# Attention steps of three units (one head pair) in place of two, one distance table, and queries scaled on the chip

## What is computed

```python
scores = scale * np.matmul(q, k.transpose(0, 1, 3, 2))
keep = is_global | is_local
dist = np.where(is_global & ~is_local, float(n_local), np.abs(rel).astype(np.float32))
bias = -slopes[:, None, None] * dist[None, :, :]
scores = np.where(keep, scores + bias, -1000000000.0)
a = np.exp(scores - max(scores))
a = a / (sum(a) + 1e-09)
x = np.matmul(a, v)
h = np.maximum(x @ w_in, 0.0)      # first product of the next layer
```

## Time and profile before

| what | value |
|---|---|
| median of 3 runs | 374.99 us |
| the profiled execution's own time | 374.08 us |
| its span, first to last instruction | 372.0 us |
| TensorE busy with matmuls | 361.2 us, 97% |
| VectorE, ScalarE, GpSimd busy | 214.7, 176.6, 76.2 us |
| TensorE in the chain that ended last | 91% of the span |
| mean granted TensorE clock | 0.998 of full |

### The profile page before, as it was taken

One profiled execution on the slowest core, in us unless ns is written; L12 is line 12 of the kernel. 1 busy time (PEld: TensorE's weight loads), 2 busy tenths in 40 slices (PEclk: granted clock), 3 DMA queues, 4 the chain that ended last, 5 costly groups with the idle time before them and its releaser, 6 DMA issues.

```text
span 372.0 us, 6143 instructions
## 1 busy us (share of the span) xinstructions
PE 361.2 (97%) x2266; PEld 323.9 (87%) x2266; DVE 214.7 (58%) x568; ACT 176.6 (47%) x450; POOL 76.2 (20%) x152
## 2 busy tenths in 40 slices
PE   6798999999999999999999999999999999999995
PEld 3466888888888899999988999998899999998884
DVE  5798586767677678679957690213863444441000
ACT  4798575674756469664255650213563111112121
POOL 4859963223233100000020210001410000000000
PEclk9999999999999999999999999999999999999999
DMA  7923323142302304131100000001141000001322
GB/s 234 409 112 130 102 86 127 35 154 84 125 37 70 131 0 169 62 112 56 58 0 0 3 0 0 2 0 45 56 168 60 0 2 0 0 2 58 114 86 90
DMA packets 11796, 27.69 MB, mean 74 GB/s; under 512 B 1520, under 2 KB 3568, under 8 KB 11760
## 3 DMA queue, kind: packets, MB, share of 16 engines
q1 hardware_dynamic: 11328, 26.95, 20.6%
q10 hardware_dynamic: 432, 0.28, 0.2%
HBM read 24.08 MB, written 3.15 MB: 73 GB/s over the span
## 4 chain that ended last, share of the span: by engine, by line
PE 91%; ACT 3%; DVE 3%; DMA 1%; POOL 1%; issue 1%; DVEq 0%; ACTq 0%
PE bank L1502 19%; PE bank L1504 19%; PE bank L1503 19%; PE bank L1471 19%; PE bank L1447 5%; PE bank L1425 4%; PE bank L1404 4%; ACT p_sb L683 2%; DMA counts<-in_n_keys 1%; DVE p_sb L1004 1%; DVE denom L1013 0%; POOL p_sb L588 0%; DVE dist L980 0%; ACT pt_sb L691 0%; POOL bias L576 0%
## 5 line engine op out<-in xcount | busy, mean ns | idle before, releaser
L1471 PE MATMUL bank<-xT,w_hi 128*128 128x384 f32 x256 | 71.3, 348 | 0.0
L588 POOL TENSOR_SCALAR p_sb<-p_sb,denom 128x256 f32<-128x256 f32 (+1 forms) x96 | 44.3, 481 | 53.3 <-DVE denom L1015 53.1
L1471 PEld LDWEIGHTS bank<-xT,w_hi 128*128 128x128 f32 x256 | 45.6, 188 | 3.5 <-issue 2.5
L683 ACT ACTIVATE p_sb<-p_sb,row_min 128x256 f32<-128x256 f32 (+1 forms) x96 | 46.3, 486 | 2.2 <-DVE row_min L1004 2.0
L1471 PE MATMUL bank<-xT,w_lo 128*128 128x384 f32 x128 | 44.6, 348 | 0.0
L1502 PE MATMUL bank<-g_hi,w_hi 128*128 128x386 f32 (+1 forms) x128 | 43.3, 338 | 0.0
L1504 PE MATMUL bank<-g_hi,w_lo 128*128 128x386 f32 (+1 forms) x128 | 43.2, 337 | 0.0
L1503 PE MATMUL bank<-g_lo,w_hi 128*128 128x386 f32 (+1 forms) x128 | 43.1, 337 | 0.0
L1041 DVE SCALAR_TENSOR_TENSOR c_sb<-h_sb,conv_sb,c_sb 128x382 f32<-128x382 f32 (+1 forms) x64 | 40.2, 628 | 2.3
L691 ACT COPY pt_sb<-bank 128x512 f32<-128x512 f32 (+1 forms) x41 | 22.6, 552 | 36.7 <-PE bank L1425 36.7
L1004 DVE CUSTOM_DVE_ANT_0 p_sb<-bank,bias 128x256 f32<-128x256 f32 (+1 forms) x96 | 33.1, 399 | 3.6 <-PE bank L1404 2.9
(11 more groups left out here) (96 smaller groups left out, 750.4 us busy)
## 6 DMA issues: line engine op xcount, KB each, us to landing
stage<-in_weights SPq DMA_DIRECT2D x17, 512.0 KB, 3.2
v_sb<-in_v SPq DMA_DIRECT2D x8, 390.0 KB, 3.1
k_sb<-in_k SPq DMA_DIRECT2D x8, 384.0 KB, 3.4
out_dram<-out_sb SPq DMA_DIRECT2D x12, 256.0 KB, 2.0
q_sb<-in_q SPq DMA_DIRECT2D x14, 192.0 KB, 2.5
k_sb<-in_k SPq DMA_DIRECT2D x6, 256.0 KB, 3.4
v_sb<-in_v SPq DMA_DIRECT2D x5, 260.0 KB, 2.7
stage_late<-in_weights SPq DMA_DIRECT2D x2, 512.0 KB, 12.5
```

The costliest lines, as they stand in the source:

```text
L588: nc.gpsimd.tensor_scalar(probs_h, probs_h, denom[:, u % SLOTS, h:h + 1], 1.0, ALU.mult, ALU.mult).then_inc(scaled, 1)
L683: nc.scalar.activation(p_sb[:, u % SLOTS, h, 0:n], p_sb[:, u % SLOTS, h, 0:n], ACT.Exp, bias=row_min[:, u % SLOTS, h:h + 1], scale=-1.0, a ...
L1471: last = nc.tensor.matmul(banks[5 + j % 3][:, 0:C], w, x, start=r == 0, stop=r == F1_GROUP - 1)
```

## The change

TensorE's loop takes one triple at a time: turn three units with 8 matmuls of `f1` behind each, then the scores of the triple two ahead in one block (three units), then `weigh` of this triple's three units. `f1` starts with triple 4, which is unit 12; 12 triples hold 24 matmuls each, again 288. The banks change: `weigh` has bank 4 alone, so `weigh` of a triple waits until `rest_of_x` of the triple before has read it; transposes have bank 3 alone after unit 12, and `pt_sb` three slots for four; `f1` has banks 6 and 7 until its last 96 matmuls. ScalarE and VectorE follow in loops by triples. VectorE copies 6 of the first 12 transposed units.

One table of distances of 640 columns stands for the eight of `bias`; it is built in three parts between the first units. The slope of a head comes in as the scale of the VectorE instruction, and so the queries are multiplied by a factor per head pair beforehand: GpSimd does that, 17 instructions, from factors that 8 short VectorE memsets write. All pieces of the weights of `f1` are split by GpSimd, 8 in place of 6.

```diff
-PT_SLOTS = 4
+PT_SLOTS = TG
-F1_FIRST = GU + 2
-F1_STEP = 8
+F1_FIRST = HP
+F1_STEP = 24
+PIECES_AFTER = {8: 1, 11: 1, 14: 2, 17: 2, 20: 2}
...
+        def score_cols(u, h):
+            p, tt = divmod(u, TG)
+            bank = banks[(2, 5)[h] if tt == 2 else (6, 7)[h] if p == 1 else h]
+            at_col = tt % 2 * 2 * P
+            return bank[:, at_col:at_col + keys(u)]
...
+            def scale_queries(pg):
+                queries = q_sb[:, pg % 2, :]
+                pool.wait_ge(q_in[pg % 2], 16 * (pg // 2 - 1))
+                nc.gpsimd.tensor_scalar(queries, queries, q_scale[:, pg % HP:pg % HP + 1], 1.0, ALU.mult, ALU.mult
+                                        ).then_inc(q_scaled, 1)
...
+            pieces = 0
             for u in range(ALL_UNITS):
                 scale_probs(u)
-                if u in (1, 2, 4, 5):
-                    table(4 + u // 2 + u // 5)
-                if PIECE_FIRST <= u < PIECE_FIRST + (NW1 - 1) * PIECES:
-                    split_piece(u - PIECE_FIRST)
+                if u == 1:
+                    scale_first_queries(2, slice(0, C), q_rest, True)
+                if u == 4:
+                    scale_first_queries(3, slice(0, C), q_rest, True)
+                for pg in range(HP, ALL_TRIPLES):
+                    if scale_unit(pg) == u:
+                        scale_queries(pg)
+                for _ in range(PIECES_AFTER.get(u, 0)):
+                    split_piece(pieces)
+                    pieces += 1
...
+            soften(0)
+            soften(1)
+            copy_pt(0)
+            soften(2)
+            for p in range(ALL_TRIPLES):
+                u = TG * p
+                for tt in range(TG):
+                    if p + 1 < ALL_TRIPLES:
+                        soften(u + TG + tt)
+                    if p >= F1_FIRST and tt == 2:
+                        relu_h(2 * (p - F1_FIRST))
+                    if u + tt > 0 and not turned_on_dve(u + tt):
+                        copy_pt(u + tt)
+                    if tt == 0 and p > 0:
+                        round_x(p - 1)
+                if p >= F1_FIRST:
+                    relu_h(2 * (p - F1_FIRST) + 1)
+            round_x(ALL_TRIPLES - 1)
...
+            for p in range(1, ALL_TRIPLES + 1):
+                u = TG * p
+                for tt in range(TG):
+                    if p + 1 < ALL_TRIPLES:
+                        bias_scores(u + TG + tt)
+                    if tt > 0 and p < HP and turned_on_dve(u + tt):
+                        take_pt(u + tt)
+                rest_of_x(p - 1)
...
+                if p > F1_FIRST:
+                    taps(*divmod(2 * (p - 1 - F1_FIRST), KF))
+                if p < HP:
+                    invert_sums(u + TG, 2)
+                    invert_sums(u + TG + 2, 1)
+                elif p + 1 < ALL_TRIPLES:
+                    invert_sums(u + TG, TG)
+                if p > F1_FIRST:
+                    taps(*divmod(2 * (p - 1 - F1_FIRST) + 1, KF))
...
             def turn_probs(u):
...
+                if u > GU and u % TG:
                     wait_pt(pe, u - 1)
-                    wait_pt(pe, u - 2)
...
+            for p in range(ALL_TRIPLES):
+                for tt in range(TG):
+                    turn_probs(TG * p + tt)
+                    if p == 0 and tt == 1:
+                        third_scores(1)
+                    if p >= F1_FIRST:
+                        for _ in range(F1_STEP // TG):
+                            f1(f1_next)
+                            f1_next += 1
+                if p + 2 < ALL_TRIPLES:
+                    scores(p + 2)
+                for tt in range(TG):
+                    weigh(TG * p + tt)
```

More of the change, by code:

```diff
@@ L382, in turned_on_dve, with copies @@
         def turned_on_dve(u):
-            return u < F1_FIRST and u % 2 == 1
+            return u < GU and (u % TG == 1 or u % TG == 2 and u // TG % 2 == 1)
+        def copies(u, on_dve):
+            return sum(turned_on_dve(i) == on_dve for i in range(u + 1))
         def wait_pt(eng, u):
             if turned_on_dve(u):
-                eng.wait_ge(pt_in_odd, u // 2 + 1)
+                eng.wait_ge(pt_in_dve, copies(u, True))
             else:
-                eng.wait_ge(pt_in, u // 2 + 1 if u < F1_FIRST else u + 1 - F1_FIRST // 2)
+                eng.wait_ge(pt_in, copies(u, False))
         def staged(n):
@@ L399, in wait_chunk @@
                 eng.wait_ge(chunk_in[n % 2], 16 * (n // 2))
+        INVERTED_ALONE = (0, 1, 2, 5, 8, 11, 14)
         def inversion(u):
[L403 to L412, removed]
+            if u < TG * (HP + 1):
+                return sum(i <= u for i in INVERTED_ALONE) - 1 + sum(i <= u for i in range(TG, TG * (HP + 1), TG))
+            return len(INVERTED_ALONE) + HP + u // TG - (HP + 1)
         def values_of(u):
@@ L1402, in score @@
-                for h in range(2):
-                    rows = slice(h * D, (h + 1) * D)
-                    last = nc.tensor.matmul(score_bank(u, h)[:, u % 2 * 2 * P:u % 2 * 2 * P + n],
-                                            queries[rows, tt * P:(tt + 1) * P], keys_t[rows, at_key:at_key + n],
-                                            start=True, stop=True)
-                return last
-            def scores(u):
-                wait_if(pe, biased, 2 * u - (4 if u < F1_FIRST else 0))
-                score(u)
-                score(u + 1).then_inc(scored, 1)
@@ L1415, in turn_probs @@
-            def turn_probs(u):
-                if u < F1_FIRST and u >= 2:
-                    wait_pt(pe, u - 2)
-                if u >= F1_FIRST:
+                else:
+                    queries, keys_t = q_sb[:, u // TG % 2, :], k_sb[:, u // TG % 2, :]
+                rows = slice(h * D, (h + 1) * D)
+                return nc.tensor.matmul(score_cols(u, h), queries[rows, tt * P:(tt + 1) * P],
+                                        keys_t[rows, at_key:at_key + n], start=True, stop=True)
@@ new lines, in score_unit, with scores @@
+            def score_unit(u):
+                score(u, 0)
+                return score(u, 1)
+            def scores(p):
+                u = TG * p
+                if p == 0:
+                    pe.wait_ge(k_first, 16)
+                elif p < HP:
+                    pe.wait_ge(k_second if p == 1 else k_rest, 16)
+                else:
+                    pe.wait_ge(k_in[p % 2], 16 * (p // 2 - 1))
+                pe.wait_ge(q_scaled, queries_scaled(p, 0))
+                if p >= 2:
+                    pe.wait_ge(biased, 2 * (TG * p - 1 if p > 2 else 2))
+                score_unit(u)
+                last = score_unit(u + 1)
+                if p < 2:
+                    last.then_inc(scored_first, 1)
+                if p != 1:
+                    third_scores(p)
@@ L1470, in f1 @@
                 x = xT[:, kappa % 2, (0, 1, 0)[part], kk, :]
-                last = nc.tensor.matmul(banks[5 + j % 3][:, 0:C], w, x, start=r == 0, stop=r == F1_GROUP - 1)
+                last = nc.tensor.matmul(h_bank(j)[:, 0:C], w, x, start=r == 0, stop=r == F1_GROUP - 1)
                 if r == F1_GROUP - 1:
```

253 lines of the change are left out of this document (101 added, 152 removed).

## The result

| what | before | after |
|---|---|---|
| median of 8 runs each | 375.12 us (373.98 to 376.02) | 373.19 us (371.74 to 374.23) |
| ratio of the times, 95% interval | | 0.9955 [0.9936, 0.9974] |
| the profiled execution: own time, span | 374.08, 372.0 us | 373.0, 371.2 us |
| TensorE busy with matmuls | 361.2 us | 359.6 us |
| VectorE, ScalarE, GpSimd busy | 214.7, 176.6, 76.2 us | 215.2, 176.8, 89.5 us |

A forecast was written before the change was run, and what follows sets the result against it. Softmax engines pace the units before the first `f1`; then TensorE's block columns and changes cost. 374.08 - 1.8 (first part) - 1.7 (filler phase) + 0.1 = 370.7 us profiled, 371.6 median; range 368.6 to 374.8.

The forecast's parts named there:

- The filler phase: First `f1` to last 96: fewer changes between blocks, net 1.7 us saved, 99.6 to 97.9.
- the change from `weigh` straight to transposes: TensorE's new block change in each triple: 0.06 us taken, 12 times, 0.7; bounds 0 and 0.10.
- The rule of the Trainium skill: Alternative price for block changes: all equally dear, 0.19 us each, 3.0 saved in place of 3.5.
- The first part: Start of the kernel up to the first `f1`: 34.56 to 32.8, 1.8 us saved.
- Then I walk the lists: Engines' instruction lists followed before the filler: pace no better, filler from unit 12 not 14, first `f1` at 32.8, 1.8 us saved.
- the loop: Before the filler: inversion, GpSimd, queries, transposes, copy, scores, `rest_of_x`, inversions; 5.2 to 5.8 us a triple.
- The start gives nothing: Rival: GpSimd's pieces and queries delay triples, first `f1` at 34.8, total 373.6; chance 0.20, shared with blocks giving nothing.
- A shorter start: Rival: shorter loop and hidden table, first `f1` at 30.1 to 31, total 368.9; chance 0.18.
- Slower: one bank for transposes: Rival: filler-phase second and third transposes wait for the copy before, 24 times 0.25 us, total 377.6; chance 0.12.
- What would show it: Signs in the trace: first `f1` at 32.8, no idle marks behind it, last 96 from 130.8, `weigh` 1.24 to 1.45.

The follow-up runs named there:

- The split of blocks: Changed kernel with four of the third unit's eight `f1` matmuls moved between scores and `weigh` of a triple: 375.43 us, ratio 1.0013 to the kernel before.
- the gaps filled: Changed kernel plus 11 matmuls on zeros into bank 4, six behind triple 1's scores, five behind the first transposes: 371.20 us, ratio 0.9909 to the kernel before.
- VectorE's order: Changed kernel with VectorE's copies of transposed units put behind all three score rows of a step: 371.92 us, ratio 0.9939 to the kernel before.
- that of the query scaling: Changed kernel with GpSimd's scaling of a triple's queries moved one unit later: 372.85 us, ratio 0.9962 to the kernel before.
- a third: Changed kernel with 11 zero matmuls, VectorE's inversions ahead of its copies in the first four triples, GpSimd's first two pieces earlier: 376.10 us, ratio 1.0034 to before.

## Why the prediction was off

**The filler phase: right.** The prediction had 99.6 become 97.9, and 0.1 for `weigh` to `f1` at the end; measured 97.7. Its parts show up one by one: `weigh` of 24 records 1.46 (its 24 x 0.053 + 0.17 is 1.44), scores of 12 records 1.49 as worked out, and for the change from `weigh` straight to transposes, in no row of before, 0.42 - 0.36 = 0.06, the value taken. That one is luck in part: the row it was taken from the earlier trace rows has an idle mark of 0.52 ahead of its transposes, so it shows no change from scores. The split of blocks gives the same price from the other side. The rule of the Trainium skill that I had set against it (TensorEngine Tiling (Array Packing), Tiling Modes: every change of mode drains the engine) made this change as dear as the others, 0.19, as I had read it; the page gives no price. The trace decides for the 0.06.

**The first part: wrong, and it is nearly the whole miss.** The step that failed is "Then I walk the lists", down to "first `f1` at 32.8. ... 1.8 saved". The walk took TensorE's blocks at prices read at the full clock and put down nothing for a fall of the clock. Its times for the softmax engines held as far as the first slow blocks: VectorE has unit 1 at 7.46 and unit 2 at 9.34, where it said 7.5 to 8.2 and 9.2 to 9.9, and its last inversion for triple 1 at 15.97 for 15.7. With the gaps filled the whole walk holds: the first `weigh` starts at 15.87 (said: near 15.8), VectorE's last inversions of triples 1 to 4 at 15.93, 20.84, 26.21 and 31.75 (said: 15.7, 20.9, 25.9, 31.6), and the first `f1` at 33.08 (said: 32.8). In the changed kernel the second of these inversions is at 22.64. What I had not asked is what TensorE does while unit 0 is early and unit 1 is not. Before, the first transposes came at 10.12 with no idle mark, because 8 records of scores stood ahead of them:

```profile
8.86 1.13 PE L1404 MATMUL bank<-k_sb,q_sb 64*128 64x256 f32 x8 [0.62 <-DVE row_min L1004]
10.12 0.59 PE L1425 MATMUL bank<-ident,p_sb 128*128 128x128 f32 x2
```

Now the first scores are done by 7.95 and the products of units 0 and 1 are not there until 9.28 and 11.03: the time gained on the keys turned into two idle marks, and these into half speed for nearly seven microseconds, at the place where the loop runs through TensorE. Of the 1.8 that I had put down, the start gives 1.5 with the clock whole (34.56 to 33.08); the low clock takes 1.8 (33.08 to 34.90).

**The sum.** Forecast for the profiled execution 370.7, measured 373.0. Of the 2.3 between them, 2.1 is the first `f1` (1.8 the low clock, 0.3 the walk), -0.3 the filler phase, 0.8 the end of the last store, and -0.3 lies around the span (1.8 us for 2.1). The median misses by less, 373.19 for 371.6, since this execution lies 0.2 under its median and not 0.9.

**The rivals.** "The start gives nothing" has the time nearly right (373.6, first `f1` at 34.8) and the mechanism wrong: no piece of GpSimd was late, since with the clock at 1.00 the same list of GpSimd gives 33.08. "A shorter start" did not come: the loop stayed at 5.38 a triple, inside the 5.2 to 5.8 of the prediction (its own terms add up to 6.0 at the upper end), and neither VectorE's order nor that of the query scaling moved it. "Slower: one bank for transposes" was real but kept away: the order scores, then `weigh`, makes ScalarE's exponentials early by the length of a `weigh`, 1.5 us.

**What would show it.** As said: `weigh` at 1.24 to 1.46, filler-phase scores at 1.49, no idle mark behind the first `f1`, nothing behind the attention changed up to the last store. Not as said: first `f1` at 34.90, outside the bounds of 31.5 to 34; the last 96 at 132.5 and not 130.8; and scores of triple 2 at 2.44. Idle marks before second and third transposes are there only ahead of the first `f1`, all for GpSimd (1.16 and 0.57 in the first triple, later 0.44 and 0.47), where they belong to the first part. VectorE's copies of units 4, 7 and 10 end idle times of 1.07, 1.38 and 1.11 us; those of 7 and 10 were released by transposes that had waited for GpSimd, that of 4 by transposes that stood behind the slow `weigh` (18.91).

**Open.** Which term keeps the triples before the filler at 5.38 was not settled: one edit left the waits as they were, one moved them, a third made a longer one. How much idling the chip allows before the clock falls was not measured either. In the kernel before TensorE is nearly idle from 14 to 15 us (0.15 busy), and the filled kernel has a mark of 1.09 (0.15 busy from 13 to 14 us), and in both the clock stays at 1.00.

## What to carry to other kernels

When a start gets shorter for one unit and not for the next, look for the hole that opens on TensorE, and fill it with matmuls on zeros: read the granted clock of the slices after every idle mark of a microsecond, because its price is paid later, in blocks that show no wait. Here a low clock cost only where TensorE was in the loop, so a warm-up should lie ahead of that place, not merely at the start. And where an engine's list mixes early work of the next step with late work of this one, the order of two blocks on another engine decides whether there is a wait; swap them in thought before moving them.

## What was new about the hardware

- TensorE's granted clock fell to 0.50 behind idle marks of 1.33 and 1.16 us, though the engine was busy between them and after them (0.58 in the slice from 9 us, 0.97 from 11 us), and was back at 0.98 in the slice from 18 us, after nearly seven microseconds at the lower level, in which TensorE was busy but for a mark of 0.57. The Trainium skill, TensorE: Matmul & The Clock Gate, Part 1, says that a monitor of the array's activity gates its clock to half; the 0.50 agrees.
- The clock column can read 1.00 while matmuls run at half speed: in the kernel without warm-up from 6 to 11 us (651 ns for a matmul of 256 columns, for 389 in the kernel before). So the durations of the rows have to be read beside the column.
- GpSimd beside VectorE's convolutions is slower. In the changed kernel (start us, duration):

```profile
49.11 1.28 POOL L619 TENSOR_SCALAR p_sb<-p_sb,denom 128x256 f32<-128x256 f32 x2 [0.83 <-DVE denom L1049]
50.38 0.87 POOL L600 TENSOR_SCALAR q_sb<-q_sb,q_scale 128x384 f32<-128x384 f32 x1
```

  A unit takes 1.28 for 0.94, and the queries 0.87 where I had reckoned 0.57 at most; at 41.68, where VectorE runs no three-operand product, they take 0.59. VectorE runs two of its three-operand products in that time (49.34 to 50.72); their mean over the kernel rose from 628 to 672 ns. The kernel before had shown it too (four products in 2.53 us at 47.71), where I hadn't looked. The Trainium skill, GPSIMD Engine Reference, Key points, says that GpSimd shares its way to SBUF with VectorE when that reads two inputs there; the rows agree. It cost nothing here, since GpSimd has slack in the filler phase.
